# Attention's transpositions and turnings back as pairs of passes in column halves

## The reference

```
# attention: B 2, H 8, S 768, D 64; 4 sink keys, window 128
scores = scale * np.matmul(q, k.transpose(0, 1, 3, 2))
keep = is_sink | in_window
a = exp(scores - max) ; a = a / (sum(a) + 1e-9)
attn = np.matmul(a, v)
# mixture: 1536 tokens of 512, 8 experts, each token goes to its best two
out[mask] += top2_w[mask, k, None] * (np.maximum(x[mask] @ w1[e], 0.0) @ w2[e])
# layer: 512 -> 2048 -> 512
h = x @ w_in ; g = h * np.tanh(softplus(h)) ; return g @ w_out
```

## Time and profile before

| | us |
|---|---|
| three runs | 769.78, 770.13, 771.22 |
| the profiled execution | 771.28 |
| its span, first to last instruction | 769.5 |
| TensorE matmuls busy | 759.8 (99% of the span) |
| VectorE, GpSimd, ScalarE busy | 508.8, 312.8, 284.6 |
| granted TensorE clock, mean share of full speed | 0.999 |

### The profile page before, as it was taken

The page is one execution under the profiler, slowest core; times in us unless marked ns, Lnnn a source line. Parts: engine busy times, 40 slices in busy tenths (PEclk is TensorE's granted clock), DMA queues, the critical chain, the costliest instruction groups (busy, mean ns, idle before and its releaser), DMA issues.

```text
span 769.5 us, 13278 instructions
## 1 busy us (share of the span) xinstructions
PE 759.8 (99%) x4238; PEld 626.1 (81%) x4239; DVE 508.8 (66%) x908; ACT 284.6 (37%) x595; POOL 312.8 (41%) x333
## 2 busy tenths in 40 slices
PE   8999999999999999999999999999999999999997
PEld 4888878888888888888888888877888888888886
DVE  5789975454545445454544445478999988888876
ACT  6988814121204003040040300355655555545443
POOL 5789839492915609247092918621110020000000
PEclk9999999999999999999999999999999999999999
DMA  5798436463622606326053624011110120010001
GB/s 187 237 300 269 146 84 190 151 204 99 223 92 98 202 31 209 114 72 228 27 189 112 213 89 124 28 55 29 29 55 1 55 56 1 0 55 1 1 1 55
DMA packets 49730, 82.93 MB, mean 108 GB/s; under 512 B 18320, under 2 KB 22480, under 8 KB 49680
## 3 DMA queue, kind: packets, MB, share of 16 engines
q1 hardware_dynamic: 31648, 33.90, 13.4%
q10 hardware_dynamic: 13600, 33.96, 13.3%
q0 software_dynamic: 4432, 14.43, 6.7%
HBM read 66.02 MB, written 16.26 MB: 107 GB/s over the span
## 4 chain that ended last, share of the span: by engine, by line
PE 90%; DVE 6%; ACT 2%; issue 1%; POOL 0%; DVEq 0%; ACTq 0%; POOLq 0%
PE bank L1459 22%; PE bank L1441 22%; PE bank L1515 14%; PE bank L1535 9%; PE bank L1540 4%; PE bank L1328 4%; PE bank L1425 4%; PE bank L1302 3%; PE bank L1311 2%; PE bank L1337 2%; PE bank L1418 2%; DVE recd L1220 1%; DVE nume L1222 1%; DVE nume L1254 1%; DVE recd L1218 1%
## 5 line engine op out<-in xcount | busy, mean ns | idle before, releaser
L601 POOL TENSOR_TENSOR wgt<-stage,wgt 128x1024 f32 (+1 forms) x64 | 151.4, 2408 | 101.7 <-ACT wgt L767 101.7
L1459 PE MATMUL bank<-wgt,hT 128*128 (+1 forms) x744 | 185.5, 398 | 0.0
L1441 PE MATMUL bank<-wgt,xT 128*128 (+1 forms) x732 | 179.6, 394 | 0.0
L1441 PEld LDWEIGHTS bank<-wgt,xT 128*128 128x128 f32 x732 | 135.1, 188 | 26.6
L1459 PEld LDWEIGHTS bank<-wgt,hT 128*128 128x128 f32 x744 | 135.2, 188 | 25.6
L767 ACT ACTIVATE wgt<-stage 128x1024 f32 (+1 forms) x64 | 61.6, 1046 | 253.7 <-PE bank L1459 251.6
L1515 PE MATMUL bank<-x2T,wgt 128*128 128x512 f32 (+1 forms) x588 | 138.6, 386 | 0.6 <-DVE nume L1222 0.5
L1515 PEld LDWEIGHTS bank<-x2T,wgt 128*128 128x128 f32 x588 | 108.5, 188 | 23.8 <-DVE nume L1222 1.8
L1535 PE MATMUL bank<-wgt,gT 128*128 128x512 f32 x384 | 97.5, 392 | 1.0 <-ACT gT L827 1.0
L1535 PEld LDWEIGHTS bank<-wgt,gT 128*128 128x128 f32 x384 | 71.3, 188 | 16.5 <-ACT gT L827 2.1
L1177 DVE TENSOR_SCALAR h<-bank 128x512 f32<-128x512 f32 x62 | 42.9, 691 | 62.0 <-PE bank L1441 61.8
(11 more groups left out here) (185 smaller groups left out, 998.9 us busy)
## 6 DMA issues: line engine op xcount, KB each, us to landing
stage<-in_moe_w ACTq DMA_DIRECT2D x48, 512.0 KB, 3.7
stage<-in_moe_w SPq DMA_DIRECT2D x16, 512.0 KB, 5.8
y_dram<-y_sb SPq DMA_DIRECT2D x31, 256.0 KB, 2.7
stage<-in_moe_w_in ACTq DMA_DIRECT2D x8, 512.0 KB, 4.7
stage<-in_moe_w_out ACTq DMA_DIRECT2D x8, 512.0 KB, 4.2
v_in<-in_v SPq DMA_DIRECT2D x8, 384.0 KB
out<-o_sb SPq DMA_DIRECT2D x12, 256.0 KB, 2.3
k_in<-in_k SPq DMA_DIRECT2D x7, 396.0 KB, 5.5
```

The costliest lines, as they stand in the source:

```text
L601: nc.gpsimd.tensor_tensor(cols(parity, 1, u * UNIT, UNIT), stage[:, u, :], cols(parity, 0, u * UNIT, UNIT).bitcast(fp32), ALU.subtract).th ...
L1441: ins = T.matmul(HA[half][:], xT[:, a, c, :], cols(par, b, c * F + half * 512, 512), start=c == 0 and n == 0, stop=c == NC - 1 and n == 2)
L1459: ins = T.matmul(YB[kk % 2][:], hT[:, a, c, :], cols(par, b, NC * UNIT + c * DM, DM), start=c == 0 and n == 0, stop=c == F // P - 1 and n ...
```

## The change

Each 128x128 transposition is written as two matmuls with the identity, each of 64 columns of the probabilities into 64 partitions of the same bank, and each turning back as two matmuls of 64 queries. Both then have the array divided as `values` has it. What is computed, the waits and the order of the units stay.

```
             def turn_probs(u):
...
                 for n, at in enumerate((0, SEC + NS, P)):
-                    ins = T.transpose(TP[b][:, n * P:(n + 1) * P], probs[m][:, at:at + P], ident[:])
+                    for part in range(0, P, D):
+                        ins = T.matmul(TP[b][part:part + D, n * P:(n + 1) * P], probs[m][:, at + part:at + part + D], ident[:], start=True, stop=True)
                 ins.then_inc(probs_transposed, 1)
...
                 pe.wait_ge(xT_copied, u + 1)
                 wait(pe, x_ready, u // 2 * 2)
-                T.matmul(back_out(u, 1)[:, 0], xT_att[u // 2 % 2][:, u % 2], turn_back[:, u // QT % PPB], start=True, stop=True).then_inc(x_turned, 1)
+                for part in range(0, P, D):
+                    ins = T.matmul(back_out(u, 1)[part:part + D, 0], xT_att[u // 2 % 2][:, u % 2, part:part + D], turn_back[:, u // QT % PPB],
+                                   start=True, stop=True)
+                ins.then_inc(x_turned, 1)
```

## The result

The kernel before took 770.67 us (median of 4 runs, 769.78 to 771.36), the changed one 781.99 us (4 runs, 781.57 to 782.44). The ratio is 1.0146, with a 95% interval from 1.0134 to 1.0157: **11.3 us slower**. The forecast was 781.5, +11.4 against the runs known then.

A forecast was written before the change was run, and what follows sets the result against it. TensorE was taken to bound attention's rounds: 20 full rounds at +0.51 us, +0.66, +0.80, -0.05 and -0.2 elsewhere, sum +11.4. From 771.28 that gives 782.7, as a median 781.5 us; 8-in-10 range 778.5 to 786.

The forecast's parts named there:

- TensorE is the bound of the rounds: Steady attention rounds: TensorE alone sets the period of about 3.7 us, so its gains or losses reach the end.
- Two passes, side by side: Transpositions: each piece becomes four passes in two pairs, 0.218 us for 0.109, +0.65 us for a round's six.
- The rule of the Trainium skill: Transpositions: transpose mode four times as fast for fp32 would mean 0.436 us a piece, near 814 us; not adopted.
- Turnings back at nothing: Turnings back: four half passes in two pairs take as long as two whole passes of 0.137 us, +0.
- A change of division costs 0.15, or 0.20 into turnings back: Switching how TensorE's array is divided costs these us; a full round goes from three changes to two, -0.15 us.
- The tail and round 46: End of attention: round 46, with two routing products, +0.80 us; the tail behind it -0.05 us.
- The five gaps: Tail: five changes of the array's division disappear, -0.85 us together.
- The beginning: Rounds 2 and 4, which wait for ScalarE: three pieces ahead of its copy cost +0.33 us each round, +0.66 together.
- No new wait: Steady rounds: later ScalarE copies and GpSimd cuts cost nothing; the rival, a new wait, +6.6 us, had chance 0.06.
- The number: Whole kernel: the terms sum to +11.4 us, giving a median of 781.5 us.

The follow-up runs named there:

- half_f16: The changed kernel with the probabilities and a copy of the identity in f16, so each half transposition is one pass: 768.16 us, ratio 0.9964.
- plain_full: The kernel before with each transposition as one plain fp32 matmul of the whole array, no halves, no transpose mode: 787.89 us, ratio 1.0220.
- full_f32r: The kernel before with each transposition as one plain whole-array matmul, probabilities and identity copy in fp32r, one pass: 772.31 us, ratio 1.0016.
- full_f16: The kernel before with each transposition as one plain whole-array matmul, probabilities and identity copy in f16, one pass: 768.51 us, ratio 0.9968.
- b_only: The kernel before with only the turnings back in column halves, transpositions still whole-array in transpose mode: 770.38 us, ratio 0.9996.
- t_only: The changed kernel with the old whole-array line for turnings back, so only transpositions are in halves: 789.97 us, ratio 1.0245.
- grouped: The changed kernel with a unit's half transpositions reordered, first column half of all three pieces, then the second: 787.57 us, ratio 1.0218.

## Why the prediction was right

- *TensorE is the bound of the rounds.* Right, and the step that carried the rest: a round got 0.50 us longer, and 20 of them are 10 of the 11.3 us. `half_f16` shows how near the other bound was: at 3.56 us a round, where it had been 3.68, VectorE is in the chain. A loss of TensorE's counted in full here, a gain did not.
- *Two passes, side by side.* Right: 576 rows, 0.109 us a pair. `plain_full` and `full_f32r` show that the second pass is the loss (with two passes 17.3 us slower, with one 1.4), `half_f16` beside `full_f16` that halves with one pass lose nothing in f16, and the values' rows were a true price for the new product. The rule of the Trainium skill by which transpose mode is four times as fast for fp32 (TensorE: Matmul & The Clock Gate, Terms) is not what the runs show for these pieces: it is twice as fast, six pieces of 128x128 in 0.71 us against 1.44 in `plain_full`.
- *Turnings back at nothing.* Right (`b_only`, 770.38 us).
- *A change of division costs 0.15, or 0.20 into turnings back.* Right in the changed kernel (0.10 in front of the values and 0.05 in their first group are gone) and in `t_only`, +0.35 a round.
- *The tail and round 46.* +0.67 in sum, forecast +0.75; the 0.05 that a change costs behind its first matmul lies behind the table's end, at the routing's product. The five gaps went as said, the last of them too (0.86 for 0.95 us to the scaling). What the prediction did not look at is VectorE, which is on the chain there for 2.4 us: it had 0.39 us of room before, and the gain used it up. That it cost next to nothing is luck; in `t_only` and `plain_full` the last turnings back take 0.54 and 0.37 us longer than in the changed kernel. This is read from the traces; no run took VectorE's work out.
- *The beginning.* +0.66 as forecast, read at the transpositions of round 6: only the first unit's pieces of each of the two rounds are ahead of ScalarE's copy, which starts 0.92 us behind the first of them, where it was 0.58 and 0.59.
- *No new wait.* Right: in rounds 8 to 44 TensorE's matmuls wait for no other engine, and ScalarE has more room than before: its copies waited 16.6 us in all for transpositions, where it was 8.6. In the round shown its wait grew by 0.34 us, where I had said 0.5 at the end of the prediction: the copy waits for the first unit alone, which is 0.33 later, as the working itself had it.
- *The number.* The terms were right to about 0.4 us in sum (+11.1 by the traces, forecast +11.4); that the medians agree to 0.1 (+11.3) is in part luck.
- Of the experiments' forecasts three were off: `grouped`, where neither theory had the lag; `plain_full` by 2.4 us, mostly since I took a pass of the whole array in plain fp32 to be as quick as one in transpose mode; and `half_f16` by 8 us from the lower of its two figures, since I let TensorE's gain through in full.

## What to carry to other kernels

Before a product changes its form to fit its neighbours, count its passes in the trace, by rows against instructions: a second pass on a full TensorE costs more (0.65 us a round) than a merged division of the array gives back (0.15). Price the new form by a row of the same shape and type; here the values' rows forecast 0.51 us more a round, and 3.70 us became 4.21. And for halves that should run beside each other, write them alternately.

## What the runs showed of the hardware

- The two column halves of the array run out of written order: in `grouped` passes of a later line start (60.37) ahead of passes of an earlier one in the other half (60.43), and the lag that arises makes each round 0.27 us longer.
- A pair of plain fp32 passes of 64 columns, side by side, takes 0.109 us; one plain fp32 pass of the whole array takes 0.112. Behind the scores the first pair loses 0.05 us, the first whole pass 0.1.
- A change of the array's division costs about 0.10 us before the next matmul starts and 0.05 after (`b_only`, and the values of the kernel before).
- A whole 128x128 piece in f16 takes 0.056 us a pass against 0.11 in fp32r, both with one pass; the row of its weight load is 98 ns long against 192 ns.
- A whole fp32 turning back behind fp32r or f16 transpositions starts slowly: 0.69 us for four passes in place of 0.64.
